# A fused attention and two-MoE kernel on one core: the hand-over from the first MoE to the second is put in another order

## The reference, cut to what matters

```python
# attention: x (4, 8, 512, 64) against 32 state rows, both ways; 544 rows of 512 per batch
x = concat([softmax(x @ state.T) @ state, softmax(state @ x.T) @ x])   # 4 x 512 + 4 x 32 = 2176 rows
# first MoE (one dense expert): mish
h = x @ w_in                              # 512 -> 2048
y = (h * tanh(softplus(h))) @ w_out       # 2048 -> 512
# second MoE: 8 experts, the best one for each row
xn = y / (norm(y) + 1e-6);  en = emb / (norm(emb) + 1e-6)
logits = xn @ en.T / tau
e = argmax(logits);  gate = softmax(logits)[e]
out = gate * (relu(y @ w1[e]) @ w2[e])    # 512 -> 1024 -> 512
```

## Time and profile before

| | us |
|---|---|
| three runs, lowest, median, highest | 715.04, 717.75, 721.53 |
| the profiled execution, its own time | 715.15 |
| its span in the profile | 713.3 |
| PE busy | 660.5 (93%) |
| PE weight loads busy | 517.4 (73%) |
| DVE busy | 443.4 (62%) |
| ACT busy | 385.4 (54%) |
| POOL busy | 51.9 (7%) |

### The profile page before, as it was taken

The page is one execution under the profiler, slowest core; times in us unless marked ns, Lnnn a source line. Parts: engine busy times, 40 slices in busy tenths (PEclk is TensorE's granted clock), DMA queues, the critical chain, the costliest instruction groups (busy, mean ns, idle before and its releaser), DMA issues. The chain is left out here.

```text
span 713.3 us, 12384 instructions
## 1 busy us (share of the span) xinstructions
PE 660.5 (93%) x4142; PEld 517.4 (73%) x4143; DVE 443.4 (62%) x688; ACT 385.4 (54%) x500; POOL 51.9 (7%) x75
## 2 busy tenths in 40 slices
PE   8786989999979999899999988979999999999995
PEld 6654766688757787676578777658888888888884
DVE  7797978979658699676668445662632451273261
ACT  3785678786557797576867334161622442162260
POOL 2000000000200002000002004000101001010101
PEclk9998999999999999999999969999999999999999
DMA  8704423100814001333001602283431270144140
GB/s 263 210 31 154 144 83 124 30 1 2 258 63 146 9 2 59 113 127 119 0 1 48 234 30 75 65 292 133 169 135 43 71 247 33 45 169 149 46 152 5
DMA packets 35350, 72.72 MB, mean 102 GB/s; under 512 B 5699, under 2 KB 5699, under 8 KB 35312
## 3 DMA queue, kind: packets, MB, share of 16 engines
q1 hardware_dynamic: 27728, 56.93, 24.4%
q0 software_dynamic: 3040, 9.13, 3.2%
q10 hardware_dynamic: 4544, 6.14, 2.8%
HBM read 60.92 MB, written 12.16 MB: 102 GB/s over the span
## 5 line engine op out<-in xcount | busy, mean ns | idle before, releaser
L611 PE MATMUL PS<-WH,gh 128*128 128x512 f32 x256 | 104.4, 408 | 4.0 <-DVE WL L1261 2.7
L611 PE MATMUL PS<-WH,gl 128*128 128x512 f32 x256 | 101.8, 398 | 0.0
L611 PE MATMUL PS<-WL,gh 128*128 128x512 f32 x256 | 101.5, 397 | 0.0
L1062 ACT ACTIVATE hh<-PS 128x512 fp32r<-128x512 f32 x42 | 22.9, 595 | 97.5 <-PE PS L715 92.5
L734 PE MATMUL PS<-WH,hh 128*128 (+1 forms) x168 | 69.2, 412 | 3.9 <-DVE hl L1481 2.6
L1471 DVE TENSOR_TENSOR WL<-raw,WH 128x1024 f32 (+1 forms) x48 | 56.4, 1222 | 25.4 <-ACT WH L1042 25.3
L1372 DVE SCALAR_TENSOR_TENSOR qq<-ww,PS 128x1024 f32<-128x1024 f32 (+1 forms) x35 | 41.6, 1187 | 44.4 <-ACT ww L959 44.2
L734 PE MATMUL PS<-WH,hl 128*128 (+1 forms) x168 | 66.8, 397 | 0.0
L734 PE MATMUL PS<-WL,hh 128*128 (+1 forms) x168 | 66.6, 397 | 0.0
L611 PEld LDWEIGHTS PS<-WH,gh 128*128 128x128 f32 x256 | 48.7, 190 | 22.4 <-issue 10.7
L975 ACT ACTIVATE ww<-ww,cst 128x1024 f32<-128x1024 f32 (+1 forms) x35 | 39.4, 1126 | 46.1 <-DVE ww L1377 46.1
(11 more groups left out here) (252 smaller groups left out, 1285.4 us busy)
## 6 DMA issues: line engine op xcount, KB each, us to landing
raw<-in_w SPq DMA_DIRECT2D x48, 512.0 KB, 4.4
raw<-in_w_in SPq DMA_DIRECT2D x36, 512.0 KB, 5.0
yg<-by_expert ACTq DMA_DIRECT2D x22, 260.0 KB, 3.1
raw<-in_w_out SPq DMA_DIRECT2D x8, 512.0 KB, 4.6
by_expert<-junk SPq DMA_DIRECT2D x1, 2080.0 KB, 9.8
wr<-in_w_in SPq DMA_DIRECT2D x4, 512.0 KB, 9.4
x_0a<-in_x SPq DMA_DIRECT2D x8, 128.0 KB, 2.8
x_0b<-in_x SPq DMA_DIRECT2D x8, 128.0 KB, 3.4
```

The source lines that it names most:

```text
L611: mm = pe.matmul(PS[:, 2 + t, :], a[:, v % 2, e, t * P:t * P + P], w[:, 8 + p, e * 512:e * 512 + 512], start=(p == 0 and e == 0 and i == 0 ...
L1062: a.activation(hh[:, 4 * j:4 * j + 4, :], PS[:, 3 + j, :].rearrange("p (k m) -> p k m", k=4), ACT.Copy).then_inc(hh_rdy, 1)
```

## The change

On ACT and DVE the split of tile 0's y (`y_hi`, `y_lo`) and the copy of batch 3's y (`y_out(3)`) come before the last split of z's operand, and one weight split and `y_out("z")` move. On PE, batch 3's tiles are turned in the order 1, 2, 0, 3 (`tile`), with halves of YB and YB(3) between them; `GT(3)` moves ahead of YB(2), `route_k(3)` behind half of PA and z's transposes. Further on, tile 1's PB changes place: before, m 0 to 3 stood ahead of `TY((0, 2))`, 4 and 5 behind it and ahead of tile 2's PA, 6 and 7 behind `TY((0, 3))`; now nothing of it stands ahead of `TY((0, 2))`, 0 and 1 behind it, and 2 to 7 behind `TY((0, 3))`. SP's wait in front of the second expert's weights goes from 48 to 64, the landing of the fourth fetch, tile 3's. The last PB is issued in two halves, the first of which waits for the first half of `hl` alone.

```diff
--- before.py
+++ after.py
@@ -254,6 +254,10 @@
         def l_bank(c):
             return {3: 2, "z": 5}.get(c, 7)
 
+
+        def tile(c, i):
+            return (1, 2, 0, 3)[i] if c == 3 else i
+
         def t_bank(c, t):
             return (6, 3, 4, 6)[t] if c == 3 else 6
 
@@ -382,7 +386,7 @@
             expert(sp.value_load(etab[0:1, E_FIRST:E_FIRST + 1], min_val=0, max_val=E - 1), 0)
             sp.wait_ge(tab_rdy, 1)
             nexp = sp.value_load(etab[0:1, E_COUNT:E_COUNT + 1], min_val=1, max_val=E)
-            sp.wait_ge(in_yg, 48)
+            sp.wait_ge(in_yg, 64)
             with sp.If(nexp > 1):
                 with sp.Fori(1, nexp) as i:
                     expert(sp.value_load(etab[0:1, bass.ds(i, 1)], min_val=0, max_val=E - 1), i * BLK)
@@ -635,11 +639,12 @@
                 if 3 in ms:
                     mm.then_inc(yb_mm, 1)
 
-            def route_t(c, t):
-                if t == 0:
+            def route_t(c, i):
+                t = tile(c, i)
+                if i == 0:
                     pe.wait_ge(y_ea, RU[c] + 1)
-                    if c != "z":
-                        pe.wait_ge(y_ed, c + 1)
+                if i == 0 and c != "z" or c == 3 and t == 2:
+                    pe.wait_ge(y_ed, c + 1)
                 if c in (0, 1) and t == 0:
                     pe.wait_ge(sc_e, 2 * c + 6)
                 if c == 2 and t == 0:
@@ -647,7 +652,7 @@
                 if c == 3 and t == 0:
                     pe.wait_ge(gz_lo, 4)
                 elif c == 3 and t == 3:
-                    pe.wait_ge(rt_e, 3 * ST + 1)
+                    pe.wait_ge(rt_e, 3 * ST + 2)
                 elif c == "z":
                     pe.wait_ge(rt_d, 2)
                 elif c != 3 and before(c) + t > 0:
@@ -656,16 +661,17 @@
                     mm = pe.transpose(PS[:, t_bank(c, t), k * P:k * P + P], rows(c)[:, t, k * P:k * P + P], ident[:])
                 mm.then_inc(rt_t, 1)
 
-            def route_l(c, t):
-                if c == 3 and t % 2 == 1:
-                    pe.wait_ge(rt_d, t // 2 + 1)
+            def route_l(c, i):
+                t = tile(c, i)
+                if c == 3 and i % 2 == 1:
+                    pe.wait_ge(rt_d, i // 2 + 1)
                 elif c == 3:
-                    pe.wait_ge(rt_e, 3 * ST + t // 2 + 1)
+                    pe.wait_ge(rt_e, 3 * ST + i // 2 + 1)
                 elif c == "z":
                     pe.wait_ge(rt_e, 3 * ST + 3)
                 else:
-                    pe.wait_ge(rt_e, before(c) + t + 1)
-                if t == 0 and c in (1, 2):
+                    pe.wait_ge(rt_e, before(c) + i + 1)
+                if i == 0 and c in (1, 2):
                     pe.wait_ge(idx_rdy, c)
                 for k in range(KT):
                     mm = pe.matmul(PS[:, l_bank(c), t * E:t * E + E], turned_to(c, t)[:, k, :], enT[:, k, :],
@@ -715,12 +721,12 @@
                         mm = pe.transpose(PS[:, 3 + j, m * P:m * P + P], hsb[:, (4 * j + m) * P:(4 * j + m + 1) * P], ident[:])
                     mm.then_inc(tr_t, 1)
 
-            def PB(t, ms=range(FT)):
+            def PB(t, ms=range(FT), by_half=False):
                 slot, o = place(t)
                 early = first(t) or second(t)
                 if first(t):
                     pe.wait_ge(y_ea, len(UNITS))
-                pe.wait_ge(hl_rdy, at(t, 2, 1 if early and ms[-1] < 4 else 2))
+                pe.wait_ge(hl_rdy, at(t, 2, 1 if (early or by_half) and ms[-1] < 4 else 2))
                 if not early:
                     pe.wait_ge(o_rdy, at(t))
                 if not first(t):
@@ -826,17 +832,20 @@
                         GT(2)
                         YB(1)
                     if p == 7:
+                        GT(3)
                         YB(2, (0, 1))
-            GT(3)
-            for t in range(ST):
-                route_t(3, t)
-            for t in range(ST):
-                route_l(3, t)
+            for i in range(3):
+                route_t(3, i)
             YB(2, (2, 3))
-            route_k(3)
+            route_l(3, 0)
+            route_l(3, 1)
+            route_t(3, 3)
             YB(3)
+            route_l(3, 2)
+            route_l(3, 3)
             PA(t0, (0,))
             route_t("z", 0)
+            route_k(3)
             PA(t0, (1,))
             TR(t0, (0,))
             route_l("z", 0)
@@ -850,14 +859,14 @@
             TR(t1, (0,))
             PB(t0, (6, 7))
             TR(t1, (1,))
-            PB(t1, (0, 1, 2, 3))
             pe.wait_ge(tab_rdy, 3)
             less4 = pe.value_load(etab[0:1, E_LESS4:E_LESS4 + 1], min_val=NT - 4, max_val=WT - 4)
             TY((0, 2))
-            PB(t1, (4, 5))
+            PB(t1, (0, 1))
             PA((0, 2))
             TY((0, 3))
-            PB(t1, (6, 7))
+            PB(t1, (2, 3))
+            PB(t1, (4, 5, 6, 7))
             TR((0, 2))
             with pe.Fori(0, less4) as i:
                 t = (i, 3)
@@ -869,7 +878,8 @@
             PA(last)
             PB(after(last, -1))
             TR(last)
-            PB(last)
+            PB(last, (0, 1, 2, 3), True)
+            PB(last, (4, 5, 6, 7))
 
         @block.scalar
         def _(act):
@@ -1008,12 +1018,13 @@
                         act.wait_ge(y_sq, before(c) + t)
                     a.activation(junk[:, 0:DM], rows(c)[:, t, 0:DM], ACT.Square, accum_out=stats(c)[:, 0, t:t + 1]).then_inc(y_sq, 1)
 
-            def turned(c, t):
-                act.wait_ge(rt_t, before(c) + t + 1)
+            def turned(c, i):
+                t = tile(c, i)
+                act.wait_ge(rt_t, before(c) + i + 1)
                 if c == 3:
                     act.wait_ge(g_lo, upto(B * PC - 1))
                 elif c != "z":
-                    act.wait_ge(rt_l, before(c) + t)
+                    act.wait_ge(rt_l, before(c) + i)
                 a.activation(turned_to(c, t), PS[:, t_bank(c, t), :].rearrange("p (k m) -> p k m", k=KT), ACT.Copy).then_inc(rt_e, 1)
 
             def gate_exp(c):
@@ -1170,18 +1181,18 @@
             whi(0, 1, 0)
             split_gz(2)
             whi(0, 2, 0)
+            y_hi(t0)
+            y_out(3)
             split_gz(3)
-            y_hi(t0)
-            whi(0, 3, 0)
-            y_out(3)
-            squares(3, (0, 1))
             turned(3, 0)
             turned(3, 2)
+            squares(3, (0, 1))
+            whi(0, 3, 0)
             squares(3, (2, 3))
+            y_out("z")
+            squares("z", (0,))
             gate_exp(3)
-            y_out("z")
             whi(0, 4, 0)
-            squares("z", (0,))
             whi(0, 5, 0)
             t1, t2 = (0, 1), (0, 2)
             relu(t0, 0)
@@ -1398,8 +1409,9 @@
                 dve.wait_ge(gz_hi, j + 1)
                 v.tensor_tensor(gzl[:, j % 2], PS[:, 6, :], gzh[:, j % 2].bitcast(F32), ALU.subtract).then_inc(gz_lo, 1)
 
-            def turned(c, t):
-                dve.wait_ge(rt_t, before(c) + t + 1)
+            def turned(c, i):
+                t = tile(c, i)
+                dve.wait_ge(rt_t, before(c) + i + 1)
                 v.tensor_copy(turned_to(c, t), PS[:, t_bank(c, t), :].rearrange("p (k m) -> p k m", k=KT)).then_inc(rt_d, 1)
 
             def y_out(c):
@@ -1659,16 +1671,16 @@
             wlo(0, 1, 0)
             lo_gz(2)
             wlo(0, 2, 0)
+            y_lo(t0)
+            y_out(3)
             lo_gz(3)
-            y_lo(t0)
-            wlo(0, 3, 0)
-            y_out(3)
             turned(3, 1)
             turned(3, 3)
+            wlo(0, 3, 0)
+            y_out("z")
             route_a(3)
             route_b(3)
             second_tile()
-            y_out("z")
             wlo(0, 4, 0)
             wlo(0, 5, 0)
             wlo(0, 6, 0)
```

## The result

The changed kernel takes 719.87 us (median of 20 runs, 716.45 to 721.74) against 717.06 (20 runs, 712.12 to 721.53): ratio 1.0043, 95% interval 1.0025 to 1.0060, so some 3.1 us slower (1.8 to 4.3 by the interval), under 1%. The profiled execution took 717.7 us with a span of 715.7, 2.4 more than before's 713.3; the sum of the prediction was +1.9.

A forecast was written before the change was run, and what follows sets the result against it. PE, busy 93% of the span, was taken as the bound. Terms -4.2 + 0.3 + 0.2 + 4.2 + 2.0 - 0.6 = +1.9 us gave 717.0 in the profile's frame, 719.6 over the median; forecast 718, range 712 to 723.

The forecast's parts named there:

- part 1: Transition: y copied earlier and tiles reordered remove PE's 4.63 us wait; idx at 424.2 to 424.4, gain 4.2 us.
- part 2: PE's longer wait for z's one-hot: PB of tile 0 starts at the low clock, +0.3 us (0 to 0.7).
- part 3: Tile 1's PB moved behind TY((0, 2)): PE stands 4.0 us there, clock may drop, TY at half speed, +0.2 us.
- part 4: SP waits for the fourth fetch: second expert's loads go out 6.3 us later, fourth weight split 4.2 us late.
- part 5: Loop's start: mostly idle PE drops the clock, 3.3 to 4.6 us at half speed, +2.0 us (0 to 2.3).
- part 6: End: the last PB's first half waits for one hl only and starts earlier, -0.6 us.
- Rival (c): Transition: the clock is lost in the mixed list of transposes, logits and YB; sum +10.1, 725.3 us, chance 0.11.
- the gain ends at POOL: Transition: PE then waits about 7.9 us for z's one-hot behind POOL's scatters, so only 4.2 us of 11 remain.
- the part given back: Second expert's loads, no longer sharing DMA with fetch and scatter, recover 2.1 of the 6.3 us shift.
- the cure of the 2.05 us wait at TY((0, 3)): PE's wait for tile 3's fetch goes, but is worth nothing because the PA behind it waits for relu.
- Rival (b): Second expert's late weights are mostly covered, about 1 us later, no clock lost: sum -3.3, 711.9 us, chance 0.12.
- Rival (a): The clock holds at the loop's start: sum -0.1, 715 to 717.6 us, chance 0.14.

The follow-up runs named there:

- e3: The kernel before with only SP's wait ahead of the second expert's weights changed, 48 to 64: 721.89 us, ratio 1.0086 to before.
- e4: e2 with z's root ahead of batch 3's scatters on POOL and tile 0's h_hi ahead of the second tile's fetch on ACT: 708.23 us, ratio 0.9901 to before.
- e5: e4 with DVE's fifth weight split moved into route_b(3)'s wait and z's route_a ahead of the two other splits: 706.09 us, ratio 0.9849 to before.
- e1: The changed kernel with SP's wait ahead of the second expert's weights back at 48: 713.85 us, ratio 0.9957 to before.
- e2: The changed kernel with SP's wait back at 48 and tile 1's PB back in its old place: 714.18 us, ratio 0.9970 to before.
- e6: The changed kernel with 15 dense matmuls nobody reads filling PE's idle time ahead of the loop's first PA: 718.05 us, ratio 1.0016 to before.

## Why the prediction came out as it did

**The terms, by the two profiles.** The last Y matmul ends 0.36 us later after the change; from it:

| term of the sum | predicted | measured |
|---|---|---|
| part 1: idx | -4.2 | -4.8 |
| not in the sum: POOL's scatters and the fetch behind them | 0 | +1.1 |
| part 2: low clock in PB(t0), up to TY(t1) | +0.3 | +0.5 |
| part 3: TY(t1) to TY((0, 2)) | +0.2 | -0.1 |
| part 4: TY((0, 2)) to the fourth split | +4.2 | +4.6 |
| fourth split to the loop's PA | 0 | 0.0 |
| part 5: clock at the loop | +2.0 | +1.3 |
| part 6: end | -0.6 | -0.6 |

With the 0.36 at the start and rounding that makes the 2.4 of the spans. That the terms add up to 2.0 where 1.9 was said is luck in part: 1.1 us that nobody had costed, 0.4 in part 4 and 0.2 in part 2 went one way, 0.6 in part 1, 0.3 in part 3 and 0.7 in part 5 the other.

**Part 1** was right in its steps: no wait for the copy, one list without a gap, idx at 424.01 (424.2 to 424.4 was said). The root of POOL took 1.93 us and ended 0.8 us later than given, still ahead of need. Rival (c), the clock lost in the mixed list, did not happen in this profile: two stretches at 1.00. The size of the gain was taken from one draw of the clock: e3 shows that the old order can lose 2.6 us less.

**That the gain ends at POOL** was right: PE waits 7.71 us where 7.9 was given, and e4 confirms the cause by removing 4.2 us of it. Not foreseen was what DVE's reordering did to POOL. The sum said that the chain was "all of them unedited", and the prediction costed wlo(0, 4) to wlo(0, 6) nowhere; but with idx earlier, the three splits, which before came one by one as ACT delivered them, stood ready in a row beside the scatters. In the timeline before:

```profile
431.67 1.23 DVE L1471 TENSOR_TENSOR WL<-raw,WH 128x1024 fp32r<-128x1024 f32 x1 [2.02 <-ACT WH L1042]
...
431.85 1.89 POOL L436 DMA_INDIRECT by_expert<-ysb,idx  x1 [0.30 <-issue]
```

The third scatter took 1.89 us beside one split, the fourth 1.26 beside the next. The last three scatters together took 4.1 us before and 5.2 after: that is the +1.1 us. In e5, where none takes over 1.04, idx to fetch is 8.3 us for 10.6, so it takes away these 1.1 and what the scatters had lost before.

**Part 4** was the decisive step and is shown twice over. The issue moved by 6.1 us against TY((0, 2)) (6.3 given), the part given back was 1.6 us in place of 2.1. That the cure of the 2.05 us wait at TY((0, 3)) is worth nothing on this path is what e1 shows: the wait is there again (0.60 behind the later PE) and the kernel is 6 us faster. Rival (b) falls with e3. That the late weights reach PE by way of the four splits and the relu is read from the waits (TR for ACT's `hsb`, 2.50 us after the change, 6.62 in e3); no run moved the splits while the weights were late. As for the Trainium skill's turn-taking between queues ("DMA: Bandwidth & Descriptors", "Queues, rings and completion order"), no run here separates the fetch's share from the loads' own; but the give-back of 1.6 us is of the size of the bytes kept out, not of the wait: from the first load's issue to the fourth split 2.9 MB moved in 10.3 us before and 2.5 MB in 8.7 us after, at 285 and 288 GB/s.

**Part 5** was right in kind, a third too large: the clock came back about 3 us into the PA, not 3.3 to 4.6. Rival (a) did not happen in this profile. The half-speed PA((0, 2)) that spoke for it did shorten the gap, to 2.50 + 1.50 with TR between, and the clock fell all the same; before held it over 2.05 + 0.56 + 1.46, and e2 lost it over a wait of 2.52 with four transposes and six matmuls behind it. In the changed kernel all three gaps cost it. What "TensorE: Matmul & The Clock Gate" of the Trainium skill ("Part 1: The HAM clock gate") says of idle time being paid again as slow matmuls, this trace agrees with, the granted clock 0.50 behind each.

**The time**: 718.0 was given, between the sum in the profile's frame (717.0) and in the median's (719.6). 719.87 was measured, and that the median's frame comes this close is luck too: the median of before's three runs was 717.75, that of twenty 717.06. The move of the medians, 3.1 us by the ratio, has an interval of 1.8 to 4.3 and so does not differ from the profiles' 2.4. Each profile is one draw: of the 23 runs of the kernel before that stand beside e1, the four slowest, 720.0 to 722.4 us, have mean granted clocks of 0.968 to 0.972, where the median of all is 0.977.

## What to carry to other kernels

A transfer that is moved behind another's landing cost the whole distance between the two issues less what the bytes gave back, here 6.1 us less 1.6; look for who stands in order behind it on every engine (here four splits ahead of a relu on ACT) before calling the disturbed transfer the problem. When a chain on one engine is brought forward, list what will now be ready on the others beside it: DVE's splits, no longer paced by ACT, slowed POOL's scatters. And where PE has been given time, ask what it waits for next: here the edit without its SP wait was worth 0.4%, and a few lines moved on POOL, ACT and DVE for that next wait brought it to 1.9%.

## What the runs showed of the hardware

An indirect DMA on POOL took 0.97 us alone and 3.26 us with three 128x1024 splits back to back on DVE, in five kernels (the changed one, e1, e2, e4, e6) to 0.01 us; a `pow` on four columns 1.04 and, beside one split, 1.93. The Trainium skill, "GPSIMD Engine Reference", section "8. Key points", has GpSimd share its SBUF interfaces with VectorE and names DVE instructions with two SBUF inputs as the ones it contends with. The split has two (`raw` and `WH`); the trace agrees in these, and e5, where two more splits ran beside scatters of 0.97 us, shows that not every overlap costs. Each slowed scatter ended 0.84 to 0.86 us after the last split beside it: before at 433.74 and 435.30 (splits to 432.90 and 434.45), after at 429.44 (428.59), e4 at 431.03 (430.17), and alike in e1, e2, e3 and e6. The scatter of e5 at 427.33 began 0.17 us ahead of its split; why the one at 428.60 was not held is open. PE's granted clock rose inside a list of eight-column matmuls and was low again in the 512-column matmuls right behind it, though PE never paused (e3: 1.00 from 420.5 to 422, 0.56 in the next 2 us).
